# Linear attention, expert layer and gated spatial layer in one kernel: gathers of x ahead of the low halves, the last expert by half blocks, the first block's gathers of y between the low halves

## Time and profile before

| | us |
|---|---|
| Median of 3 runs | 406.55 (405.27 to 407.39) |
| Profiled execution, its own time | 407.85 |
| Span of its instructions | 406.1 |
| TensorE busy | 369.0 |
| GpSimd busy | 189.4 |
| VectorE busy | 203.1 |
| ScalarE busy | 141.6 |
| Mean granted TensorE clock | 0.971 |

### The profile page before, as it was taken

How to read it: one execution, slowest core, us unless ns; L and a number is a source line. 1 busy time by engine, 2 the same in 40 slices (tenths; PEclk the granted TensorE clock), 3 DMA queues, 4 the chain that set the end, 5 groups by cost and what they waited for, 6 DMA issues and landing times.

```text
span 406.1 us, 6119 instructions
## 1 busy us (share of the span) xinstructions
PE 369.0 (91%) x2481; PEld 348.0 (86%) x2481; DVE 203.1 (50%) x353; ACT 141.6 (35%) x215; POOL 189.4 (47%) x145
## 2 busy tenths in 40 slices
PE   5889999955879998999999999775999999999997
PEld 5789899944669997989899999554999998899996
DVE  7798889426593548562434522124505532803530
ACT  1113223212341656373544505034621224731122
POOL 2796899401948376959586508175500000510000
PEclk9999999975898999999999999998999999999999
DMA  7979979510193958595865810153000011000002
GB/s 266 384 262 382 389 272 363 192 41 0 40 326 111 301 174 310 182 340 177 295 226 163 275 75 2 41 141 93 2 0 0 2 57 62 0 2 0 2 19 97
DMA packets 30671, 61.58 MB, mean 152 GB/s; under 512 B 2417, under 2 KB 17650, under 8 KB 30642
## 3 DMA queue, kind: packets, MB, share of 16 engines
q1 hardware_dynamic: 23634, 47.80, 33.9%
q10 hardware_dynamic: 5216, 7.87, 5.3%
q0 software_dynamic: 1792, 5.51, 4.5%
HBM read 51.33 MB, written 9.83 MB: 151 GB/s over the span
## 4 chain that ended last, share of the span: by engine, by line
PE 66%; DMA 13%; POOL 9%; DVE 4%; issue 3%; ACT 3%; SPq 1%; POOLq 0%; DVEq 0%
PE bank L1204 16%; PE bank L1206 16%; PE bank L1205 16%; POOL w_l L392 8%; DMA x_in<-x_dram,inv 7%; PE bank L1138 4%; PE bank L1095 2%; DMA kT<-k_feat 2%; DMA raw<-w_in 2%; PE bank L1159 2%; PE bank L1134 2%; PE bank L1118 2%; POOL x_in L558 2%; PE bank L1151 1%; DMA y_dram<-y_out 1%
## 5 line engine op out<-in xcount | busy, mean ns | idle before, releaser
L392 POOL TENSOR_TENSOR w_l<-raw,w_h 128x1536 fp32r<-128x1536 f32 x24 | 87.8, 3671 | 34.0 <-ACT w_h L387 33.8
L1204 PE MATMUL bank<-xT_h,w_h 128*128 128x256 f32 x192 | 54.4, 283 | 1.7 <-DVE xT_l L768 1.7
L1205 PE MATMUL bank<-xT_l,w_h 128*128 128x256 f32 x192 | 54.3, 283 | 0.0
L1206 PE MATMUL bank<-xT_h,w_l 128*128 128x256 f32 x192 | 54.3, 283 | 0.0
L387 ACT ACTIVATE w_h<-raw 128x1536 fp32r<-128x1536 f32 x32 | 47.0, 1483 | 18.8 <-DVE inv L751 10.2
L597 POOL TENSOR_TENSOR v_l<-v_nrm,v_h 128x512 fp32r<-128x512 f32 x12 | 15.5, 1291 | 64.4 <-ACT v_h L1051 64.4
L1204 PE MATMUL bank<-w_h,hT_h 128*128 128x384 f32 x128 | 44.0, 344 | 0.0
L1205 PE MATMUL bank<-w_l,hT_h 128*128 128x384 f32 x128 | 43.5, 340 | 0.0
L1206 PE MATMUL bank<-w_h,hT_l 128*128 128x384 f32 x128 | 43.5, 339 | 0.0
L995 ACT ACTIVATE hT_h<-bank 128x512 fp32r<-128x512 f32 x32 | 18.9, 593 | 58.1 <-PE bank L1206 44.4
L1204 PEld LDWEIGHTS bank<-xT_h,w_h 128*128 128x128 f32 x192 | 36.8, 191 | 1.9 <-DVE xT_l L768 1.9
(11 more groups left out here) (188 smaller groups left out, 842.2 us busy)
## 6 DMA issues: line engine op xcount, KB each, us to landing
raw<-w SPq DMA_DIRECT2D x28, 768.0 KB, 6.3
vN<-v_tok SPq DMA_DIRECT2D x6, 576.0 KB, 5.4
rT<-r_feat SPq DMA_DIRECT2D x6, 512.0 KB, 6.7
kT<-k_feat SPq DMA_DIRECT2D x6, 512.0 KB, 8.1
kN<-k_tok SPq DMA_DIRECT2D x6, 512.0 KB, 7.6
raw<-w ACTq DMA_DIRECT2D x4, 768.0 KB, 10.7
y_dram<-y_out SPq DMA_DIRECT2D x16, 192.0 KB
rN<-r_tok SPq DMA_DIRECT2D x6, 384.0 KB, 5.7
```

Source lines behind the costliest of these rows:

```text
L392: eng.tensor_tensor(low, raw_of(n), high.bitcast(F32), ALU.subtract).then_inc(s_low[kind], 1)
L1204: mm(dst, left_h, right_h, start=(k == 0), stop=False)
L1205: mm(dst, left_h, right_l, start=False, stop=False)
L1206: return mm(dst, left_l, right_h, start=False, stop=(k == last_k))
```

## The change

1. GpSimd issues the gather of expert e + 1 first and then makes the three low halves of e + 1, where two of them stood before the gather.
2. `down` of the last expert takes all 8 steps of half 0 and then those of half 1. The first gathers of y wait for the stores of half 0, and for those of half 1 of the last expert only if that expert has more than 128 tokens in block 0 (`y1_need`, two small VectorE operations in the run at expert 0). All gathers still wait for VectorE's release.
3. Three gathers of y are issued at once (`AHEAD`); gathers 3, 4 and 5 follow low halves 0, 1 and 2 of v; gathers 6 to 11 follow low half 5 and the last store.
4. The constant `eps` is set early and a square root of it is taken by ScalarE before the gated layer; `stay_warm` has 2 products in place of 6.

```diff
+AHEAD = 3
...
             gather_x(0)
-            for n in range(first[1], first[1] + 2):
-                make_low(pool, n)
             for e in range(E):
                 if e + 1 < E:
                     pool.wait_ge(s_xt, e + 1)
                     gather_x(e + 1)
-                    make_low(pool, first[e + 1] + 2)
+                    for n in range(first[e + 1], first[e + 1] + 3):
+                        make_low(pool, n)
                 else:
                     for n in range(n_moe, len(parts)):
                         make_low(pool, n)
-                if e + 2 < E:
-                    for n in range(first[e + 2], first[e + 2] + 2):
-                        make_low(pool, n)
...
-            for t in range(2):
-                pool.wait_ge(s_yout[t], 16 * E)
+            need = pool.value_load(y1_need[0:1, 0:1], min_val=16 * (E - 1), max_val=16 * E)
+            pool.wait_ge(s_yout[0], 16 * E)
+            pool.wait_ge(s_yout[1], need)
+            pool.sem_inc(s_passed, 1)
             pool.wait_ge(o_yout, more * 32 + 32)
             pool.sem_inc(s_passed, 1)
...
-            for c in range(NC):
-                gather_y(c)
-            for n in range(NC):
+            def low_v(n):
                 q, c = n % 2, n % NCB
                 pool.wait_ge(g_vh, n + 1)
                 nc.gpsimd.tensor_tensor(v_l[:, c, :], v_nrm[q][:, :], v_h[:, c, :].bitcast(F32),
                                         ALU.subtract).then_inc(g_vl, 1)
+
+            for c in range(AHEAD):
+                gather_y(c)
+            for n in range(NCB):
+                low_v(n)
+                if n + AHEAD < NCB:
+                    gather_y(n + AHEAD)
+            pool.wait_ge(s_yout[1], 16 * E)
+            for c in range(NCB, NC):
+                gather_y(c)
+            for n in range(NCB, NC):
+                low_v(n)
...
+            nc.vector.memset(eps[:, :], 1e-6).then_inc(s_eps, 1)
...
+            chain.link(nc.vector.tensor_scalar(spill[:, :], upto[0:1, E - 1, NCB - 1:NCB], float(P), None, ALU.is_gt))
+            nc.vector.tensor_scalar(y1_need[:, :], spill[:, :], 16.0, 16.0 * (E - 1), ALU.mult, ALU.add)
...
-            nc.vector.memset(eps[:, :], 1e-6).then_inc(s_eps, 1)
...
             act.wait_ge(s_eps, 1)
+            nc.scalar.activation(root[:, :], eps[:, :], ACT.Sqrt, bias=eps[:, 0:1])
...
-                for k in range(KF):
-                    if k % 4 == 0:
+                steps = [(k, t) for k in range(KF) for t in range(2)]
+                if e == E - 1:
+                    steps = [(k, t) for t in range(2) for k in range(KF)]
+                for k, t in steps:
+                    if t == 0 and k % 4 == 0:
                         pe.wait_ge(s_low[("w2a", "w2b")[k // 4]], e + 1)
-                    if k % 2 == 0:
+                    if t == 0 and k % 2 == 0:
                         pe.wait_ge(s_hl, 4 * e + k // 2 + 1)
-                    for t in range(2):
-                        done = down_matmuls(k, t, w2_h, w2_l)
-                        if k == KF - 1:
-                            done.then_inc(s_down, 1)
+                    done = down_matmuls(k, t, w2_h, w2_l)
+                    if k == KF - 1:
+                        done.then_inc(s_down, 1)
...
-            stay_warm(6, b_bc[:, 0:512])
+            stay_warm(2, b_bc[:, 0:512])
```

More of the change, by code:

```diff
@@ L141, in build @@
         y_pos = sb("y_pos", [P, NC], U32)
+        spill = sb("spill", [1, 1])
+        y1_need = sb("y1_need", [1, 1], I32)
         edge_no = sb("edge_no", [P, E])
@@ L233, in build @@
         eps = sb("eps", [P, 1])
+        root = sb("root", [P, 1])
         out_sb = [sb(f"out_sb{q}", [P, D]) for q in range(2)]
```

## The result

The changed kernel takes 424.0 us (median of 4 runs, 422.28 to 425.49); the kernel before takes 406.06 beside it. The ratio is 1.044, 95% interval 1.0398 to 1.0482: slower by 17.9 us, where 13.5 were forecast. The forecast time was 420.0, and 424.0 lies in the predicted range of 410 to 428.

The account below looks back on a forecast made before the run. TensorE bounds the kernel, busy 369 of 406.1 us, so only its standstills count. Terms +0.8 + 7.7 + 5 = +13.5 us on 407.85 give 421.3; the profiled run stood 1.3 above the median, hence 420.0, range 410 to 428.

Parts of the forecast that it names:

- Part 3: Block 0's value stage: three standstills of 5.9 us before batches 2, 3, 4; +7.7 us including the earlier start, clock +5.
- the row of 3.03: Value stage: a gather takes 3.03 us from issue to landing, by the profile; taken for the chain.
- the shorter 2.45: Value stage: the skill's estimate for a gather's landing, 2.45 us; the three steps would be 1.7 us shorter.
- Rival C: Value stage: a stall of the old kind, ScalarE taking batch 1 late, comes on top; about 425 us, chance 0.10.
- Part 2: Last down projection to first value batch: first gather 1.9 us after it instead of 6.0, gain 4.1 us.
- cost nothing: Before the value stage: four warm-up products fewer, an earlier memset and the early Sqrt table load cost no time.
- Rival D: Before the value stage: the early start doesn't happen, release behind the second store; +4.1, 424 us, chance 0.03.
- Part 1: Experts' stage: expert 0 loses 4.2 us, later experts' waits for x go, -3.4 us; sum +0.8 us.
- then waits once per low half: Expert 0: VectorE's small operations wait for GpSimd's low halves one by one; first hidden low half 4.2 us later.
- Rival A: Expert 0: VectorE's small operations do not wait; experts' stage -8.4 us, result about 411 us, chance 0.10.
- B: Experts' stage and earlier start outweigh the value stage's new chain, which ends faster: 402.8 us, chance 0.03, level 0.04.

Follow-up runs that it names:

- part 1 alone: The kernel before, with only GpSimd's order in the experts' stage changed (gather first, then three low halves): 412.73 us against 405.47, ratio 1.0159.
- part 2 alone: The kernel before, with only the last expert taken by halves, six gathers before the last store's wait, 2 warm-up products: 400.63 us, ratio 0.9868.
- the kernel with the semaphore: Changed kernel, six gathers at once, small operations late; at expert 0 one low half, gather, then GpSimd waits for VectorE's low half: 392.42 us, ratio 0.9596.
- the kernel with four warm-up products: The kernel with the semaphore, with 4 warm-up products in place of 2: 389.06 us, ratio 0.9562 to the kernel before.

## Why the prediction was right, and where its terms were off

**Part 3, right, with its place and its size.** The chain ran as written, three standstills of 5.76 to 5.87 us for 5.9. The gathers landed in 2.98 to 3.09 us, so the row of 3.03 was right and the shorter 2.45, which the prediction set beside it as an estimate, did not come. The clock cost a little more than was taken: steps between the starts of batches 2, 3 and 4 are 10.4 and 10.25 us, for 8.3 at full clock, about 2 us for each batch instead of 1.7. Over the whole stage it cost 6.1 us (37.5, less 14.0 for a stage at full clock, less 17.4 of standstill) where +5 was taken. The stage came out 0.7 longer than forecast. What I mis-sized more was what it replaces. I counted the 4.26 us standstill before batch 3 as a property of the kernel before. Neither the profile with part 1 alone, with the same burst of twelve gathers, nor the one with part 2 alone shows it. If most executions of the kernel before lack it, part 3 costs more than the difference of the two profiles says, and alone it did: 20.8 us. Rival C, a stall of that kind on top, did not occur in any later profile. Its cause stays open; the burst of gathers alone isn't it. The profile of the kernel before shows one thing more. The transposes of chunk 3 end at 273.55 by TensorE's record, and ScalarE takes them only at 279.08:

```profile
273.06 0.49 PE L1297 MATMUL bank<-ident,XG 128*128 128x128 f32 x3
...
279.08 0.49 ACT L1026 ACTIVATE x2T_h<-bank 128x384 fp32r<-128x384 f32 x1 [1.65 <-remote]
```

ScalarE took batch 1 3.0 us after its record, where in the eleven other profiles it was less than 0.1 us. Batch 3 needs the chunk that ScalarE and VectorE then finish. So by these rows the standstill came from a late release of what TensorE had finished, and not from a gather that TensorE waited for.

**Part 2, right.** -3.8 in the stage table for -4.1, and -4.8 by time alone. The first gather left 0.92 us after the last down product, earlier than my 1.9, because the store of half 0 had landed long before (it took 1.8 us, where the sum had 4.42) and only VectorE's release was awaited. Its landing took 4.22 us instead of 2.96, which gave the rest back. First the row of GpSimd, then the piece of the chain:

```profile
262.40 0.96 POOL L590 DMA_INDIRECT XG<-y_dram,y_pos  x1 [3.19 <-DVEq L853]
```

```profile
262.40 4.22 DMA XG<-y_dram,y_pos
```

In all nine kernels with part 2 the first gather took 3.7 to 4.6 us to land, in the three without it 3.0 to 3.1. In the nine the last store was still on its way (in the changed kernel issued at 262.10, 0.3 us before the gather); that this is the reason was not tested. That fewer warm-up products "cost nothing" isn't confirmed: see the profiles counted above. Rival D (released only behind the second store) is out.

**Part 1, the wrong step.** The place was right, and by the table the sum nearly so (+1.6 for +0.8), but "then waits once per low half" is what failed. So did the start: VectorE's own low half was to get in first and the run to begin at 108.7, 1.6 us after the first up product; in the changed kernel it began at 121.81, 12.4 us after it. In the changed kernel a single operation of VectorE waited for three low halves in a row; with part 1 alone several waited for one each and one for two, and the whole is 7.3 us by time. So the term is not one number: 18.4 and 23.9 us to the first down product in the two profiles, against 12.9. For the later experts the gain was 4.7 us rather than 3.4: from the start of the last up product to that of the first down product experts 1 to 6 took 8.9 us before and 4.2 after, and the rows of waits count only 3.5 us of that. The Trainium skill ("SBUF — State Buffer", section "SBUF: two separate sides") has the port pair go to whoever starts first, for the whole instruction. The traces agree on whole instructions: with part 1 alone three small operations of 0.2 to 0.4 us lasted 3.49 to 3.52 us, one GpSimd low half each. They also show that an operation that waits can be passed by the other engine's next instructions too, 12.57 us behind three of them. Why it was passed in one kernel and not in the other stays open; the traces differ in that it began 0.40 us after the issue of a gather in the first and 0.05 us after in the second. Rival A, no waiting at all, is out, and with it B, whose gain rested on A.

The three parts alone add up to +7.3 - 4.8 + 20.8 = +23.3 us, and together they cost 17.9. The difference of 5.4 is about that between the two courses of expert 0 (23.9 against 18.4 us to the first down product), though no run separates it from part 4 and from what the parts do to each other. So there is luck in the number. Part 1 was 6.5 us too low by its own run and part 3 4.0 (+16.8 on its own: 27.1 + 5 - 15.3). Had the course of part 1 alone come with the whole change, an estimate from these runs is 424.0 + 5.4 = 429.4 us, above the predicted range.

## What to carry to other kernels

Before an issue is moved behind another operation in a queue, follow what that operation waits for on each engine, in queue order: here a gather for chunk 3 came to depend on batch 1, and TensorE needed it before batch 2. A prefetch needs a lead of at least its whole chain of waits divided by the time of a step (5.9 by 2.4 us is 2.5 steps, so three more than the three that were there). And when one of two engines that share a port is freed from a wait, its instructions follow each other without a gap: see who stands beside it with short operations, and give that engine its turn by a semaphore or move its operations to where the other is idle.

## What was not expected of the hardware

- VectorE's tensor_tensor of 1.75 us lasted 12.55 to 12.60 us in five profiles, begun 0.4 us after GpSimd had started issuing a gather that three tensor_tensor followed. Begun 0.05 us after, it ran at once (109.39 and 109.34, part 1 alone); in the kernel with the semaphore it began 0.39 us after the gather and also ran at once, with no tensor_tensor queued behind.
- A cast of 1 x 5 numbers, one input only, lasted 6.94 us beside two tensor_tensor of GpSimd (6.80 us together, part 1 alone), where it took 0.16 us otherwise.
- The issue of a gather by GpSimd took 2.30 us in place of 0.95 while VectorE ran a tensor_tensor of two SBUF tiles (107.99 to 110.29 in the kernel with four warm-up products, VectorE from 107.72 to 109.47).
- ScalarE's table load took 1.28 us (253.81 in the changed kernel), and the square root began at 255.10: no further delay was seen. In the kernel before they were 1.28 us (271.94) and 273.23.
